# A first pass that goes by pairs of steps, and a SyncE that waits for keys before it loads the fifth weights

## The chip, the cores and the metric

One core of a Trainium2 chip. The metric is the device time of one execution, in microseconds (us); less is better. Five engines work beside each other: PE (TensorE: matmuls), DVE (VectorE), ACT (ScalarE), POOL (GpSimd) and SP (SyncE, which here only starts DMA transfers). ACT starts some transfers as well. Each engine takes its instructions in order, and they wait for each other through semaphores.

## The reference, cut to what matters

```python
# per batch (4) and head (8), D = 48, 768 time steps
cur = outer(u * k_t, v_t)
y_t = r_t @ (state + cur)
state = w_t[:, None] * state + outer(k_t, v_t)
# then, for 3072 tokens of width 384
h = x @ w_in                      # 384 -> 2048
g = h * clip(h + 3, 0, 6) / 6
x = g @ w_out                     # 2048 -> 384
xn = x / rms(x) * rms_g
out = (silu(xn @ w_gate) * (xn @ w_val)) @ w_out2
```

## The kernel before

The attention runs in chunks of 64 time steps, in 24 sets g (a chunk of two batches each). Each set has a cumulative product of decays by a scan (`prep_scan`), its reciprocal (`prep_inv`, in two parts), the scaled keys (`prep_k`) and receptances (`prep_r`), scores, a masked product with the values (`outputs`), new state sums (`sums`) and the part from the older state (`across`). The weights of the first expert layer come from memory as fp32, and are split into a hi part (ACT, `split_up`, L491) and a lo part (POOL, `split_up`, L927), for products of three matmuls in the fast format; the down products of the first pass use the raw fp32 weights (`down_raw`, L1104).

A pass e handles 512 tokens (the passes 0 and 1 handle 256 each) in NF1 = 16 steps f. In step f PE makes `up(e, f)`: nine matmuls into one of two PSUM banks. ACT (`up_gate`, L536) and DVE (`hidden`, L789) turn the bank into g, and PE later multiplies g by the down weight (`down`, L1094), two steps behind. `up(f)` waits until hidden(f - 2) has freed its bank (s_g) and, in pass 0, for the lo part of weight f (s_wloU). The attention of the coming sets lies in these steps by a table written by hand: `half_a` (L260) for pass 0, `cycles` for the others. A set has four phases: MEET (scores of set g + 1, outputs, sums and across of set g), PREP, INV1 and INV2. All engines walk the same table. The order on each engine is the order of the Python program:

- SP (L414 to L453) loads dec, rkn, rkt and weights in a fixed order, with waits before each that frees its buffer. After `load_rk(2)` it goes straight on to the weights 4 and 5 (`FIRST_UP` = 4), then `load_dec(3)`, `load_rkn(3)`, `load_rk(3)`.
- ACT (L665 to L693) copies and fills the bonus of sets 0 and 1 into the attention matrix, copies keys, splits the first weights and copies x1 (`x1_hi`, L524), which waits for `outputs`. In pass 0 each step evacuates `up`, then does attention, a split and the fill of bonus 2.
- DVE (L885 to L910) prepares sets 0 and 1, masks scores, makes x1's lo part, `update_state(0)`, `prep_scan(2)`; then 16 steps of `hidden` and attention.
- POOL (L1012 to L1029): products `rk_mul` and `prep_r` of sets 0 and 1, the lo splits, and `rku_mul(2)` between the second and the third split.
- PE (L1277 to L1294): warm-up matmuls `busy`, bonuses, scores, keys, sums, outputs of sets 0 and 1, then the passes in `run1` (L1219). A semaphore's name tells the maker: s_ki scaled keys, s_kiT transposed keys, s_g g, p_y outputs.

`meet(e, f, g)` on PE is, for a set with state: `scores(g + 1)` (L1129), `outputs(g)` (L1158, from set 2 on), a wait for hidden(f - 1), `sums(g)` (L1150) into two PSUM banks (one of them the up bank that is free) and `across(g)` (L1186, from set 2 on).

Of the kernel before, what the change touches and what calls it, by code (L numbers as in the profile page):

```python
# [40 lines left out]
NF1, NF2 = F1 // P, F2 // P  # L41
# [15 lines left out]
FIRST_UP = 4  # L57
# [10 lines left out]
def build(nc, decT, rkT, valN, rkN, u, u_heads, w_in, w_out, w_gate, w_val, w_out2, rms_g, out, x2_dram):  # L68
    with ExitStack() as ctx:
# [94 lines left out]
        def sum_bank(g, b):  # L164

            if b == 0:
                return ps_c
            return ps_o[2] if g == 0 else ps_h[g == 1]

        s_val0, s_val3, s_rkt, p_bn, s_half, s_last = (sem(n) for n in ("s_val0", "s_val3", "s_rkt", "p_bn", "s_half", "s_last"))  # L170
        ldD = [sem(f"ldD{i}") for i in range(2)]
# [46 lines left out]
        def has_state(g):  # L218

            return g < GROUPS - SETS  # L220
# [12 lines left out]
        def sums_read(eng, g):  # L233

            need(eng, s_state, STATE_INCS * g + 2)
# [14 lines left out]
        MEET, PREP, INV1, INV2 = range(4)  # L250

        def cycles(c):

            steps = {0: [(INV2, c * B - 1)]}
            for b in range(B):
                for phase in (MEET, PREP, INV1, INV2):
                    steps.setdefault(4 * b + 1 + phase, []).append((phase, c * B + b))
            return steps

        half_a = {4: [(MEET, 1)], 6: [(PREP, 1)], 7: [(INV1, 1)], 8: [(INV2, 1)],  # L260
                  9: [(MEET, 2)], 10: [(PREP, 2)], 11: [(INV1, 2)], 12: [(INV2, 2)],
                  13: [(MEET, 3)], 14: [(PREP, 3)], 15: [(INV1, 3)]}

# [83 lines left out]
        def _(sp):  # L347
# [7 lines left out]
            def load_rk(g):  # L355

                need(sp, s_ki, g - 1)
                need(sp, s_rd, g - 1)
                if PLACED <= g < 2 * PLACED:
                    sp.wait_ge(s_rkt, g - 1)  # L360
                for j in (1, 0):
                    sp.dma_start(rkt[HI2 * j:HI2 * j + D, slot(g), :, :, :, :], rkT[g // SETS, g % SETS, j, 0:D]).then_inc(ldR[slot(g)], 16)
# [57 lines left out]
            load_rkn(2)  # L420
            load_dec(2)
            load_rk(2)
            for f in range(FIRST_UP, FIRST_UP + 2):
                load_up(sp, f)
                load_dn(sp, f - 2)
# [54 lines left out]
        def _(act):  # L480
# [10 lines left out]
            def split_up(f):  # L491

                act.wait_ge(ldUp[f], 16)
                act.activation(w_up[:, f, 0, :], raw_up[:, f, 1, :], ACT.Copy).then_inc(s_whiU, 1)
# [6 lines left out]
            def fill_bonus(g, part):  # L501

                q = slot(g)
                if part == 0:
                    act.wait_ge(s_bonus, g + 1)
                    need(act, p_y, g - 1)
                for j in range(2):
                    for p in range(2 * part, 2 * part + 2):
                        last = act.activation(att[:, q, j, p, :], diag[:, :], ACT.Copy, scale=bonus[:, q, 2 * p + j:2 * p + j + 1])
                        last.then_inc(s_fill, 1)  # L510
# [160 lines left out]
                    copy_keys(0)  # L671
            for g in range(2):
                keep_last(g)
            split_up(0)
            x1_hi(0, 0)
            split_up(1)
            x1_hi(1, 0)
            copy_keys(1)
            for f in range(2, FIRST_UP):
                split_up(f)  # L680
            for f in range(NF1):
                up_gate(0, f)
                for phase, g in half_a.get(f, ()):
                    if (phase, g) != (MEET, 1):
                        attention(phase, g, 0)
                if f + FIRST_UP < NF1:
                    split_up(f + FIRST_UP)
                if f in (1, 2):
                    fill_bonus(2, f - 1)
                if f in (1, 4):  # L690
                    keep_last((2, 3)[f // 4])
                if f >= LATE:
                    split_dn(f - LATE)  # L693
# [15 lines left out]
        def _(dve):  # L709
            def prep_scan(g):  # L710

                q = slot(g)
                landed(dve, ldD, g, 2)
                need(dve, s_ki, g - 1)
                need(dve, s_rd, g - 1)
                need(dve, s_last, g - 1)
                dve.tensor_tensor_scan(*(t.rearrange("p a b t -> p (a b t)") for t in (
                    cum[0:DP, q, :, :, :], dec[0:DP, q, :, :, :], first1[0:DP, :, :, :])), 1.0,
                                       ALU.mult, ALU.add).then_inc(s_cum, 1)
# [11 lines left out]
            def prep_k(g):  # L731

                q = slot(g)
                landed(dve, ldR, g, 2)
                dve.wait_ge(s_inv, PAIRS * (g + 1))
                dve.tensor_tensor(*(t.rearrange("p a b t -> p (a b t)") for t in (
                    ki[0:DP, q, :, :, :], rkt[0:DP, q, 1, :, :, :], ki[0:DP, q, :, :, :])), ALU.mult).then_inc(s_ki, 1)
# [31 lines left out]
            def sum_bonus(g):  # L769

                dve.wait_ge(s_rku, g + 1 - PLACED)
                need(dve, s_fill, H * (g - 1))
                dve.tensor_reduce(bonus[:, slot(g), :], rkn[:, slot(g), 0, :].rearrange("p (h d) -> p h d", h=H),
                                  AX_X, ALU.add).then_inc(s_bonus, 1)
# [118 lines left out]
            for g in range(2):  # L893
                x1_lo(g, 0)
            update_state(0)
            prep_scan(2)
            for f in range(NF1):
                hidden(0, f)
                if f == 0:
                    sum_bonus(2)  # L900
                if f < 2:
                    prep_inv(2, f)
                if f == 2:
                    prep_k(2)
                if f == 3:
                    prep_scan(3)
                for phase, g in half_a.get(f, ()):
                    attention(phase, g, 0)
                if f in (4, 5):
                    prep_inv(3, f - 4)  # L910
# [15 lines left out]
        def _(pool):  # L926
# [27 lines left out]
            def rk_mul(g):  # L954

                landed(pool, ldR, g, 2)
                r_in, k_in = (rkt[0:DP, g, i, :, :, :].rearrange("p a b t -> p a (b t)") for i in range(2))
                pool.tensor_tensor(rk_t[g][0:DP, :, :], r_in, k_in, ALU.mult).then_inc(s_rkt, 1)

            def prep_r(g):  # L960

                q = slot(g)
                landed(pool, ldR, g, 2)
                pool.wait_ge(s_cum, g + 1)
                need(pool, p_y, g - 1)
                pool.tensor_tensor(*(t.rearrange("p a b t -> p (a b) t") for t in (
                    rd[0:DP, q, :, :, :], rkt[0:DP, q, 0, :, :, :], cum[0:DP, q, :, :, 0:T])), ALU.mult).then_inc(s_rd, 1)
# [43 lines left out]
            pool.memset(val3[:, :, :, :, :], 0.0).then_inc(s_val0, 1)  # L1011
            rk_mul(0)  # L1012
            prep_r(0)
            prep_r(1)
            rk_mul(1)
            for f in range(2):
                split_up(f)
            pool.wait_ge(ldU, 16 * PB)
            rku_mul(2)
            for f in range(2, FIRST_UP):  # L1020
                split_up(f)
            prep_r(2)
            for f in range(NF1):
# [17 lines left out]
        def _(pe):  # L1041
# [40 lines left out]
            def up(e, f, par):  # L1082
                need(pe, s_g, e * NF1 + f - 1)
                if e == 0:
                    pe.wait_ge(s_wloU, f + 1)
                if (e, f) == (0, 1):
                    pe.wait_ge(s_kiT, 2)
                dst = ps_h[f % 2][:, tokens(e)]
                if f == 0:
                    first_hidden(dst, w_up[:, f], par, tokens(e), B // 2 if e == 0 else B * e).then_inc(p_up, 1)  # L1090
                else:
                    into_hidden(dst, w_up[:, f], par, tokens(e)).then_inc(p_up, 1)
# [114 lines left out]
            def meet(e, f, g):  # L1207

                if g + 1 < GROUPS:
                    scores(g + 1)  # L1210
                if g >= PLACED:
                    outputs(g)
                if has_state(g):
                    pe.wait_ge(s_g, e * NF1 + f)
                    sums(g)
                if g >= PLACED:
                    across(g)

            def run1(e, par, steps, norm=None):  # L1219

                for f in range(NF1):
                    for phase, g in steps.get(f - 1, ()):
                        if phase == MEET and has_state(g):
                            sums_read(pe, g)
                    if e in (1, 2) and f == 0:
                        down(e - 1, NF1 - 2)
                    up(e, f, par)
                    for phase, g in steps.get(f, ()):
                        if phase == MEET:
                            meet(e, f, g)  # L1230
                        if phase == INV1 and has_state(g + 1):
                            keys(g + 1)
                    if (e, f) == (0, 2):
                        sums_read(pe, 0)
                    if f >= 2:
                        down(e, f - 2)
                    elif e and (f == 1 or e > 2):
                        down(e - 1, NF1 - 2 + f)
                    if norm:
                        norm(f)  # L1240
# [41 lines left out]
            scores(0)  # L1282
            keys(0)
            busy(3)
            pe.wait_ge(s_bonus, 1)
            sums(0)
            bonuses(1)
            busy(4)
            scores(1)
            outputs(0)  # L1290
            outputs(1)
            pe.wait_ge(s_bonus, PLACED)
            keys(1)
            run1(0, 0, half_a)  # L1294
            run1(1, 0, cycles(1))
            for c in range(2, NCH):
                run1(c, (c - 1) % 2, cycles(c))
# [82 lines left out]
```

## Time and profile before

| | us |
|---|---|
| median of 3 runs | 935.19 (935.14 to 936.35) |
| the profiled execution | 934.01 |
| its span in the trace | 932.3 |
| PE busy | 919.8 (99%) |
| DVE, ACT, POOL busy | 518.8, 362.0, 293.2 |

The profile is of one execution, 1.2 us below the median of the runs. Times in it count from the start of the span. A row of the timeline gives the start, the length, the engine, the line of the kernel, the operation, what it writes and reads, how many instructions were merged, and in brackets how long the engine had been idle before it and what released it. An SPq row is a DMA issue by SP. The clock column (PEclk) is the share of TensorE's full clock that was granted, 1.00 for 2.4 GHz and 0.50 for 1.2 GHz.

### The profile page before, as it was taken

To read this page: it belongs to the slowest core of one execution; us is meant where nothing else is said; L and a number is where in the kernel's file an instruction comes from. 1 tells how busy PE (TensorE), PEld (TensorE's weight loads), DVE (VectorE), ACT (ScalarE), POOL (GpSimd) and SP (SyncE) were. 2 spreads that over 40 slices of the span, in tenths; PEclk is the share of its full clock that TensorE was granted. 3 is DMA by queue.
4 is the path that set the end of the run, shared out by engine and by line. 5 is a ranking of instruction groups with operands and counts; after the bars stand their busy time and mean duration, and the time that the engine had idled before them with its cause. 6 is when DMAs were issued, how large, how long until landed. Compare 5 with 4: busy or idle time off the path is not lost.

```text
span 932.3 us, 17546 instructions
## 1 busy us (share of the span) xinstructions
PE 919.8 (99%) x7064; PEld 772.9 (83%) x7064; DVE 518.8 (56%) x752; ACT 362.0 (39%) x786; POOL 293.2 (31%) x244
## 2 busy tenths in 40 slices
PE   7999999999999999999999999999999999999998
PEld 6899988888888888888888888888888888888887
DVE  5998976666656666314874553553463373363332
ACT  4556554454444444336563123123223223223212
POOL 3888645454445445324341011011011001101000
PEclk9999999999999999999999999999999999999999
DMA  9774442233223321014321010000010001000000
GB/s 257 231 207 128 118 130 61 69 98 96 66 62 106 80 72 52 20 40 134 88 88 38 1 35 34 1 34 34 0 34 35 1 25 44 0 1 34 1 1 34
DMA packets 33008, 60.40 MB, mean 65 GB/s; under 512 B 6112, under 2 KB 19936, under 8 KB 32928
## 3 DMA queue, kind: packets, MB, share of 16 engines
q1 hardware_dynamic: 27104, 50.82, 18.9%
q10 hardware_dynamic: 5824, 8.47, 3.1%
q8 instruction: 56, 0.92, 0.4%
q14 instruction: 24, 0.20, 0.1%
HBM read 47.66 MB, written 9.44 MB: 61 GB/s over the span
## 4 chain that ended last, share of the span: by engine, by line
PE 96%; issue 1%; DVE 1%; ACT 1%; POOL 1%; SPq 0%; DMA 0%; DVEq 0%; ACTq 0%; POOLq 0%
PE acc L1076 35%; PE bank L1047 12%; PE bank L1049 12%; PE bank L1048 12%; PE pair L1049 5%; PE pair L1048 5%; PE pair L1047 5%; PE acc L1110 2%; PE pair L1129 1%; PE pair L1186 1%; PE pair L1158 1%; PE bank L1150 1%; PE bank L1065 1%; PE acc L1275 1%; PE bank L1139 1%
## 5 line engine op out<-in xcount | busy, mean ns | idle before, releaser
L1076 PE MATMUL acc<-gs,w_dn 128*128 128x512 f32 (+1 forms) x1512 | 357.0, 382 | 0.2 <-issue 0.2
L1076 PEld LDWEIGHTS acc<-gs,w_dn 128*128 128x128 f32 x1512 | 273.0, 188 | 54.0 <-issue 0.3
L943 POOL TENSOR_TENSOR gs<-act_g,gs 128x512 fp32r<-128x512 f32 (+1 forms) x96 | 121.7, 1268 | 205.3 <-ACT gs L549 205.1
L1047 PE MATMUL bank<-xs,w_up 128*128 128x512 f32 (+1 forms) x459 | 172.0, 375 | 1.5 <-POOL w_up L930 1.4
L1049 PE MATMUL bank<-xs,w_up 128*128 128x512 f32 (+1 forms) x459 | 169.0, 368 | 0.0
L1048 PE MATMUL bank<-xs,w_up 128*128 128x512 f32 (+1 forms) x459 | 169.0, 368 | 0.0
L799 DVE SCALAR_TENSOR_TENSOR act_g<-act_u,bank 128x512 f32<-128x512 f32 (+1 forms) x112 | 67.5, 602 | 137.9 <-ACT act_u L541 137.8
L867 DVE TENSOR_TENSOR act_u<-act_u,bank 128x512 f32<-128x512 f32 x72 | 49.5, 688 | 146.8 <-ACT act_u L611 146.8
L541 ACT ACTIVATE act_u<-bank,half 128x512 f32<-128x512 f32 (+1 forms) x112 | 70.1, 626 | 154.1 <-PE bank L1049 144.5
L615 ACT ACTIVATE gs<-act_g 128x512 fp32r<-128x512 f32 x72 | 45.5, 632 | 155.9 <-DVE act_g L873 155.9
L611 ACT ACTIVATE act_u<-bank 128x512 f32<-128x512 f32 x72 | 43.1, 598 | 149.0 <-PE bank L1049 149.0
L1047 PEld LDWEIGHTS bank<-xs,w_up 128*128 128x128 f32 x459 | 86.4, 188 | 16.8 <-issue 1.6
L1048 PEld LDWEIGHTS bank<-xs,w_up 128*128 128x128 f32 x459 | 86.5, 188 | 14.8
L1049 PEld LDWEIGHTS bank<-xs,w_up 128*128 128x128 f32 x459 | 86.4, 188 | 14.6
L989 POOL TENSOR_TENSOR xs<-ntmp,xs 128x512 fp32r<-128x512 f32 x18 | 26.1, 1448 | 225.8 <-ACT xs L574 225.8
L729 DVE RECIPROCAL ki<-cum 112x128 f32<-112x128 f32 x96 | 84.2, 921 | 0.8
L549 ACT ACTIVATE gs<-act_g 128x512 fp32r<-128x512 f32 (+1 forms) x96 | 57.2, 596 | 65.9 <-DVE act_g L799 65.3
L873 DVE TENSOR_TENSOR act_g<-act_u,pair 128x512 f32<-128x512 f32 x72 | 49.6, 688 | 51.9 <-PE pair L1049 51.2
L877 DVE TENSOR_TENSOR gs<-act_g,gs 128x512 fp32r<-128x512 f32 x72 | 55.3, 768 | 36.8 <-ACT gs L615 36.3
L1047 PE MATMUL pair<-xs,w_up 128*128 128x512 f32 x144 | 56.0, 389 | 0.0
L1048 PE MATMUL pair<-xs,w_up 128*128 128x512 f32 x144 | 56.0, 389 | 0.0
L1049 PE MATMUL pair<-xs,w_up 128*128 128x512 f32 x144 | 56.0, 389 | 0.0
(121 smaller groups left out, 1121.2 us busy)
## 6 DMA issues: line engine op xcount, KB each, us to landing
rkn<-in_rkN SPq DMA_DIRECT2D x22, 384.0 KB, 4.2
rkt<-in_rkT SPq DMA_DIRECT2D x44, 192.0 KB, 3.7
val<-in_valN SPq DMA_DIRECT2D x22, 256.0 KB, 3.0
x<-x_dram SPq DMA_DIRECT2D x6, 768.0 KB, 4.3
dec<-in_decT SPq DMA_DIRECT2D x46, 97.5 KB, 2.3
x_dram<-xo SPq DMA_DIRECT2D x5, 768.0 KB, 4.1
out<-xo SPq DMA_DIRECT2D x5, 768.0 KB, 3.3
raw_dn<-in_w_out SPq DMA_DIRECT2D x14, 192.0 KB, 5.2
```

Of the source, the lines that this page charges most:

```text
L541: act.activation(act_u[:, f % 2, tok], ps_h[f % 2][:, tok], ACT.Relu, scale=1.0 / 6.0, bias=half[:, 0:1]).then_inc(s_u, 1)
L549: act.activation(gs[:, f % GRING, 0, tok], act_g[:, f % 2, tok], ACT.Copy).then_inc(s_ghi, 1)
L729: dve.reciprocal(ki[0:DP, q, p, :, :], cum[0:DP, q, p, :, 1:T1]).then_inc(s_inv, 1)
L799: dve.scalar_tensor_tensor(out=g_of(e, f), in0=act_u[:, f % 2, tok], scalar=1.0, in1=ps_h[f % 2][:, tok], op0=ALU.min, op1=ALU.mult).then_ ...
L867: dve.tensor_tensor(act_u[:, f % 2, :], act_u[:, f % 2, :], ps_h[f % 2][:, :], ALU.mult).then_inc(s_silu, 1)
L873: dve.tensor_tensor(act_g[:, f % 2, :], act_u[:, f % 2, :], ps_v[f % 2][:, :], ALU.mult).then_inc(s_h, 1)
L877: dve.tensor_tensor(gs[:, f % GRING, 1, :], act_g[:, f % 2, :], gs[:, f % GRING, 0, :].bitcast(F32), ALU.subtract).then_inc(s_hlo, 1)
L943: pool.tensor_tensor(gs[:, f % GRING, 1, tok], act_g[:, f % 2, tok], gs[:, f % GRING, 0, tok].bitcast(F32), ALU.subtract).then_inc(s_glo, 1)
L1047: pe.matmul(dst, w_hi, x_hi, start=first, stop=False)
L1048: pe.matmul(dst, w_hi, x_lo, start=False, stop=False)
L1049: last = pe.matmul(dst, w_lo, x_hi, start=False, stop=end)
L1076: last = pe.matmul(ps_o[m][:, tok], w[:, wp, m * P:(m + 1) * P], gs[:, f % GRING, xp, tok], start=f == 0 and a == 0, stop=f == nf - 1 and ...
```

## The change

SP waits for the scaled keys of set 1 (s_ki 2) before it starts the loads of weights 4 and 5 and all behind them. Pass 0 gets a PE function of its own: two ups, then (from the second pair on) two downs; the meeting of set 1 moves from step 4 to step 5, so that meetings are at 5, 9 and 13 and the sums use the same up bank each time. In the start, `bonuses(1)` goes ahead of `sums(0)` on PE; on POOL `rk_mul(1)` goes ahead of `prep_r(1)`, behind a wait for the scan of set 1, and three splits instead of two stand ahead of `rku_mul(2)`; on ACT the second split goes ahead of `x1_hi(0)` and the third between the two `x1_hi`; bonus 2 is filled in steps 2 and 3 instead of 1 and 2. On DVE `prep_scan(2)` goes behind `hidden(0)` and `sum_bonus(2)` from step 0 to step 2.

```diff
--- before.py
+++ after.py
@@ -165,7 +165,7 @@
 
             if b == 0:
                 return ps_c
-            return ps_o[2] if g == 0 else ps_h[g == 1]
+            return ps_o[2] if g == 0 else ps_h[0]
 
         s_val0, s_val3, s_rkt, p_bn, s_half, s_last = (sem(n) for n in ("s_val0", "s_val3", "s_rkt", "p_bn", "s_half", "s_last"))
         ldD = [sem(f"ldD{i}") for i in range(2)]
@@ -257,7 +257,7 @@
                     steps.setdefault(4 * b + 1 + phase, []).append((phase, c * B + b))
             return steps
 
-        half_a = {4: [(MEET, 1)], 6: [(PREP, 1)], 7: [(INV1, 1)], 8: [(INV2, 1)],
+        half_a = {5: [(MEET, 1)], 6: [(PREP, 1)], 7: [(INV1, 1)], 8: [(INV2, 1)],
                   9: [(MEET, 2)], 10: [(PREP, 2)], 11: [(INV1, 2)], 12: [(INV2, 2)],
                   13: [(MEET, 3)], 14: [(PREP, 3)], 15: [(INV1, 3)]}
 
@@ -420,6 +420,7 @@
             load_rkn(2)
             load_dec(2)
             load_rk(2)
+            sp.wait_ge(s_ki, 2)
             for f in range(FIRST_UP, FIRST_UP + 2):
                 load_up(sp, f)
                 load_dn(sp, f - 2)
@@ -671,12 +672,13 @@
                     copy_keys(0)
             for g in range(2):
                 keep_last(g)
-            split_up(0)
+            for f in range(2):
+                split_up(f)
             x1_hi(0, 0)
-            split_up(1)
+            split_up(2)
             x1_hi(1, 0)
             copy_keys(1)
-            for f in range(2, FIRST_UP):
+            for f in range(3, FIRST_UP):
                 split_up(f)
             for f in range(NF1):
                 up_gate(0, f)
@@ -685,8 +687,8 @@
                         attention(phase, g, 0)
                 if f + FIRST_UP < NF1:
                     split_up(f + FIRST_UP)
-                if f in (1, 2):
-                    fill_bonus(2, f - 1)
+                if f in (2, 3):
+                    fill_bonus(2, f - 2)
                 if f in (1, 4):
                     keep_last((2, 3)[f // 4])
                 if f >= LATE:
@@ -893,14 +895,14 @@
             for g in range(2):
                 x1_lo(g, 0)
             update_state(0)
-            prep_scan(2)
             for f in range(NF1):
                 hidden(0, f)
                 if f == 0:
-                    sum_bonus(2)
+                    prep_scan(2)
                 if f < 2:
                     prep_inv(2, f)
                 if f == 2:
+                    sum_bonus(2)
                     prep_k(2)
                 if f == 3:
                     prep_scan(3)
@@ -1011,13 +1013,14 @@
             pool.memset(val3[:, :, :, :, :], 0.0).then_inc(s_val0, 1)
             rk_mul(0)
             prep_r(0)
+            pool.wait_ge(s_cum, 2)
+            rk_mul(1)
             prep_r(1)
-            rk_mul(1)
-            for f in range(2):
+            for f in range(3):
                 split_up(f)
             pool.wait_ge(ldU, 16 * PB)
             rku_mul(2)
-            for f in range(2, FIRST_UP):
+            for f in range(3, FIRST_UP):
                 split_up(f)
             prep_r(2)
             for f in range(NF1):
@@ -1216,25 +1219,39 @@
                 if g >= PLACED:
                     across(g)
 
-            def run1(e, par, steps, norm=None):
-
-                for f in range(NF1):
-                    for phase, g in steps.get(f - 1, ()):
-                        if phase == MEET and has_state(g):
-                            sums_read(pe, g)
-                    if e in (1, 2) and f == 0:
-                        down(e - 1, NF1 - 2)
-                    up(e, f, par)
-                    for phase, g in steps.get(f, ()):
-                        if phase == MEET:
-                            meet(e, f, g)
-                        if phase == INV1 and has_state(g + 1):
-                            keys(g + 1)
-                    if (e, f) == (0, 2):
+            def step(e, f, par, steps):
+
+                for phase, g in steps.get(f - 1, ()):
+                    if phase == MEET and has_state(g):
+                        sums_read(pe, g)
+                up(e, f, par)
+                for phase, g in steps.get(f, ()):
+                    if phase == MEET:
+                        meet(e, f, g)
+                    if phase == INV1 and has_state(g + 1):
+                        keys(g + 1)
+
+
+            def first_pass():
+
+                for f in range(0, NF1, 2):
+                    step(0, f, 0, half_a)
+                    step(0, f + 1, 0, half_a)
+                    if f == 2:
                         sums_read(pe, 0)
                     if f >= 2:
+                        down(0, f - 2)
+                        down(0, f - 1)
+
+            def run1(e, par, steps, norm=None):
+
+                for f in range(NF1):
+                    if f == 0 and e < 3:
+                        down(e - 1, NF1 - 2)
+                    step(e, f, par, steps)
+                    if f >= 2:
                         down(e, f - 2)
-                    elif e and (f == 1 or e > 2):
+                    elif f == 1 or e > 2:
                         down(e - 1, NF1 - 2 + f)
                     if norm:
                         norm(f)
@@ -1282,16 +1299,16 @@
             scores(0)
             keys(0)
             busy(3)
+            bonuses(1)
             pe.wait_ge(s_bonus, 1)
             sums(0)
-            bonuses(1)
             busy(4)
             scores(1)
             outputs(0)
             outputs(1)
             pe.wait_ge(s_bonus, PLACED)
             keys(1)
-            run1(0, 0, half_a)
+            first_pass()
             run1(1, 0, cycles(1))
             for c in range(2, NCH):
                 run1(c, (c - 1) % 2, cycles(c))
```

## Rows read from the trace of the kernel before

**Rows 1.** The page: part 1 (engines) and part 3 (DMA queues).
```profile
PE 919.8 (99%) x7064; PEld 772.9 (83%) x7064; DVE 518.8 (56%) x752; ACT 362.0 (39%) x786; POOL 293.2 (31%) x244
...
q8 instruction: 56, 0.92, 0.4%
```

**Rows 2.** Busy time by stretch: PE, PEld, DVE, ACT, POOL, PEclk, DMA share, GB/s.
```profile
13.10:19.10 6.00, 4.01 (x124) 3.69 (x125) 4.02 (x6) 3.51 (x15) 1.51 (x2) 1.00 1.07 274
...
17.70:21.70 4.00, 0.00 (x0) 0.00 (x0) 0.73 (x1) 0.92 (x5) 0.99 (x1) 0.97 1.07 299
...
21.70:24.90 3.20, 3.15 (x59) 2.92 (x59) 1.26 (x3) 1.81 (x4) 1.60 (x2) 0.50 1.06 244
...
28.30:69.90 41.60, 41.56 (x549) 38.32 (x550) 38.44 (x58) 23.76 (x70) 34.66 (x31) 1.00 0.73 215
...
46.00:46.70 0.70, 0.70 (x5) 0.60 (x4) 0.70 (x1) 0.70 (x5) 0.70 (x1) 1.00 0.27 89
```

**Rows 3.** Timeline of PE, 20 to 29 us: start, length, engine, line, what.
```profile
21.75 0.37 PE L1165 MATMUL pair<-att,val 64*64 64x64 f32 x3 [4.07 <-issue]
...
28.34 0.36 PE L1047 MATMUL bank<-xs,w_up 128*128 128x256 f32 x1 [1.44 <-POOL w_up L930]
```

**Rows 4.** DMA queues in 19.1 to 20.2 us: packets, MB, share.
```profile
q8 instruction: 1, 0.02, 6.2%
```

**Rows 5.** The chain that ended last, in order of time: start, length, what.
```profile
13.59 0.22 PE bank L1150
...
35.01 0.45 PE bank L1150 x28
...
35.46 1.49 PE acc L1110 x6
...
38.03 1.30 PE acc L1110 x6
...
47.89 0.62 PE pair L1129 x32
...
67.27 2.61 PE acc L1110 x12
```

**Rows 6.** Timeline of SP, a DMA issue.
```profile
13.31 0.43 SPq L320 DMA_DIRECT2D raw_up<-in_w_in  x1
```

**Rows 7.** DMA queues in 46.6 to 47.7 us.
```profile
q8 instruction: 1, 0.02, 5.7%
```

**Rows 8.** Timeline of DVE, 15 to 36 us.
```profile
15.17 0.69 DVE L736 TENSOR_TENSOR ki<-rkt,ki 112x512 f32<-112x512 f32 x1
...
25.20 1.23 DVE L717 TENSOR_TENSOR_SCAN cum<-dec,first 112x520 f32<-112x520 f32 x1
...
26.38 0.42 DVE L799 SCALAR_TENSOR_TENSOR act_g<-act_u,bank 128x256 f32<-128x256 f32 x1
...
27.27 0.55 DVE L773 TENSOR_REDUCE bonus<-rkn 128x8 f32<-128x384 f32 x1 [0.47 <-POOL rkn L952]
...
27.74 0.94 DVE L729 RECIPROCAL ki<-cum 112x128 f32<-112x128 f32 x1
...
28.88 2.56 DVE L729 RECIPROCAL ki<-cum 112x128 f32<-112x128 f32 x3
...
33.05 2.69 DVE L717 TENSOR_TENSOR_SCAN cum<-dec,first 112x520 f32<-112x520 f32 x1
```

**Rows 9.** Timeline of ACT, 22 to 33 us.
```profile
22.32 0.49 ACT L530 ACTIVATE xs<-pair 128x384 fp32r<-128x384 f32 x1 [3.71 <-PE pair L1165]
...
30.07 0.51 ACT L494 ACTIVATE w_up<-raw_up 128x384 fp32r<-128x384 f32 x1
...
30.48 1.05 ACT L509 ACTIVATE att<-diag,bonus 128x64 f32<-128x64 f32 x4
...
32.06 0.47 ACT L541 ACTIVATE act_u<-bank,half 128x256 f32<-128x256 f32 x1 [0.53 <-PE bank L1049]
```

**Rows 10.** Timeline of POOL.
```profile
24.26 1.02 POOL L950 TENSOR_TENSOR rkn<-rkn 128x384 f32<-128x384 f32 x1
```

More of the change, by code:

```diff
@@ L1217, in meet @@
                     across(g)
+            def step(e, f, par, steps):
[13 more added lines that the diff above has]
+                    if f == 2:
+                        sums_read(pe, 0)
+                    if f >= 2:
+                        down(0, f - 2)
+                        down(0, f - 1)
             def run1(e, par, steps, norm=None):
                 for f in range(NF1):
-                    for phase, g in steps.get(f - 1, ()):
-                        if phase == MEET and has_state(g):
-                            sums_read(pe, g)
-                    if e in (1, 2) and f == 0:
+                    if f == 0 and e < 3:
                         down(e - 1, NF1 - 2)
-                    up(e, f, par)
-                    for phase, g in steps.get(f, ()):
-                        if phase == MEET:
-                            meet(e, f, g)
-                        if phase == INV1 and has_state(g + 1):
-                            keys(g + 1)
-                    if (e, f) == (0, 2):
-                        sums_read(pe, 0)
+                    step(e, f, par, steps)
                     if f >= 2:
                         down(e, f - 2)
-                    elif e and (f == 1 or e > 2):
+                    elif f == 1 or e > 2:
                         down(e - 1, NF1 - 2 + f)
```

## The prediction

> **What bounds the kernel now.** I read the page first: TensorE (PE) is busy 99% of the span [rows 1], so time can only come out of a hole in PE or of work taken from it, and the change takes no matmul away. The stretches come next [rows 2]. From 28.3 to 69.9 us, the rest of the first pass, PE works 41.56 of 41.60 us. Before it stand 4 us without any PE work (17.7 to 21.7) and 3.2 us at a granted clock of 0.50, the lower level, 1.2 GHz; the clock fell after PE had stood still for nearly four microseconds.
>
> PE's own timeline names the hole [rows 3]: it stops inside `outputs(0)`, with three matmuls of line 1165 to go, for 4.07 us, and the releaser is "issue". No semaphore is waited for there. The instruction queue of PE moved 56 packets of 16 KB [rows 1]; 7064 matmuls and as many weight loads over 56 are some 252 instructions a packet. One such packet moved in 19.1 to 20.2 [rows 4], and 1.5 us after its end PE went on. So I read the hole as a late block of instructions. PE had run some 456 by then; it enters the block before the missing one near instruction 200, which is the start of `sums(0)` at 13.59 [rows 5], and that is when the next can be asked for. It moved 5.5 us later, with the DMA engines full (1.07 from 13.1 to 19.1 [rows 2]). By 13.3 SP had issued u_b, rkn, dec and rkt, then from 13.31 on [rows 6] weights, dec(3), rkn(3) and rkt(3). At the other end of the scale a packet went in 46.6 to 47.7 [rows 7], just after the DMA share had been 0.27 [rows 2]: there PE has no pause that the views put forward.
>
> **Part 1: SP waits for s_ki 2, then loads the fifth weights.** `prep_k(1)` ends at 15.86 [rows 8], so the loads from 13.31 start some 2.6 us later. Queued behind the wait on SP: up weights 4 and 5 and down weights 2 and 3, dec, rkn and rkt of set 3, then up 6 and down 4, up to `load_val(2)`, where SP stood anyway until `outputs(0)` was done, at about 22; that slack covers the shift. Late next is the fifth hi/lo split, which PE wants only at step 4. Cost: nothing. Gain: if packets are served in the order in which they are asked for, the fetch now finds only what was issued by 13.3. From 13.1 to 19.1 the engines moved 274 GB/s [rows 2], 1.64 MB. What SP had issued by 13.3 and had hardly begun is u_b, rkn, dec and rkt of set 2, by their shapes in the code 1.15 MB, 4.2 us at that rate: they are through at 17.3, and the packet can go then instead of at 19.1. So the pause ends near R = 19.9 in place of 21.75, and a little sooner as the bonus stands earlier: I take R = 19.8; bounds 17.7 (no pause) and 21.75. A pause of 2.1 us need not drop the clock; I take full clock.
>
> **Part 2: bonuses(1) first on PE, rk_mul(1) first on POOL, splits regrouped.** The bonus moves ahead of `sums(0)` and `fill_bonus(1)` ends about 1.3 us earlier, but that lies in front of the pause and is worth nothing while the pause stands. The third weight's lo part no longer waits behind `rku_mul(2)`: the 1.44 us that PE waited for it ahead of 28.34 [rows 3] goes, if nothing else is late. I price that with the next part, since something else is.
>
> **Part 3: pairs of steps.** On PE they save nothing: a down is 1.30 between two ups, and two downs side by side took 2.61 [rows 5]. They ask for more sooner: up 3 comes before any down, and the meeting at 5 needs `hidden(4)` only one up after up 4.
>
> **Part 4: the scan of set 2 goes behind hidden(0).** This is where I expect the start's gain to be eaten. VectorE (DVE) does, in order: scan(2), a reciprocal, hidden(1), three reciprocals, hidden(2), sum_bonus(2); then ScalarE (ACT) fills, evacuates up 3, splits a weight, fills again, evacuates up 4; then DVE does hidden(4), for which `sums(1)` waits. From the scan's end [rows 8, 9]: 0.94 + 0.40 + 2.56 + 0.38 + 0.55 = 4.83; 1.05 + 0.47 + 0.51 + 1.05 + 0.47 = 3.55; 0.4; ten hand-overs at 0.04: together 9.2. Then the sums and downs 2 and 3: before, sums at 35.01 to the end of down 2 at 36.95 and 1.30 for down 3, 3.24 [rows 5]. So six ups and four downs are done at scan end + 12.5 (0.05 for the hand-over). Before, that point was 38.03 + 1.30 = 39.33 [rows 5]. Gain = 26.8 - scan end.
>
> When does the scan end? Before, `hidden(0)` began 4.63 after R (26.38 - 21.75) [rows 3, 8]. With PE at full clock some 1.4 of its 3 us in between go (half of the rest of the outputs and of up 0), and the split that ACT now does between the two x1 copies adds 0.5 [rows 9]: R + 3.7, ended at R + 4.1. POOL meanwhile: x1_hi(0) at R + 0.4 and 0.49 long, the split 0.51, then lo(2) 1.0 to R + 2.45, two multiplications at 1.02 to R + 4.5, lo(3) to R + 5.5 [rows 9, 10]. Scans took 1.23 and 2.69 us [rows 8]; the long one began in a stretch of POOL instructions back to back. So the scan either goes in at R + 4.5 (end R + 5.65) or behind the next split (R + 6.65). With R = 19.8 it ends at 25.45 to 26.45: gain 1.35 to 0.35, I take the middle, 0.9. PE alone would be there 3 us sooner, so the freed PE time mostly turns into waiting for s_g at up 3, up 5 and the sums of the meeting.
>
> **Part 5: the meeting at 9.** It stands 12 PE instructions (one down) earlier in the stream. A block boundary lies just ahead of it now, the next just before its end: a meeting is four groups of 32 weight loads and matmuls like the scores' 0.62 us [rows 5], some 2 us, and a fetch takes 1.1 us on its queue and 1.5 until PE goes on [rows 3, 4], plus its start. Before, the packet in 46.6 to 47.7 [rows 7] came just in time. Now the distance is 2.3 us in place of 2.7: cost 0.15 at least; up to 1.8 if the fetch falls behind the decays and rkt loads, as the first one did. I take 0.3. The bank swap (`sum_bank` to bank 0) and sums_read cost nothing: two downs, 2.6 us, lie between the meeting and the next up.
>
> Behind the first pass the instructions are the same, and PE is 99% busy, so the shift is carried to the end. Sum: 0.9 - 0.3 = 0.6 us off the profiled execution: 934.01 to 933.4. The median of the runs is 935.19, 1.2 above the profiled one; so 934.6.
>
> **Rivals.** (A) The fetch is in time and there is no pause. For it: the moved bonus and the wait both help, and one fetch at low DMA load was prompt. Against it: the 1.15 MB of u_b, rkn, dec and rkt issued by 13.3 are still moving until about 17. POOL then binds: from 17.7 three splits at 1.0, two multiplications, a split and the scan: its end is 24.95, or 23.9 if it goes ahead of the last split. Gain 1.85 to 2.9, less 0.3: 933.1 (932.6 to 933.7). Should the DVE chain be shorter than I make it, PE's own bound adds up to 1.5 more, 931.8.
>
> (B) Slower: the fetch does not queue behind SP's loads, and the delay does not move it; R stays at 21.75. With the clock at half, hidden(0) ends at 26.8 as before, but the scan, which was over at 26.43, now ends at 28.05 to 28.5. Gain 26.8 - 28.3 = -1.5, and 0.3 at the meeting: 937.0 (936.3 to 938.7). It decides from R above 20.9, where 26.8 - (R + 6.15) falls below -0.3. For it: that the packet waited behind data is read off one fetch. Against it: the 5.5 us under load, and no visible delay at 46.6.
>
> The Trainium skill, DMA: Bandwidth & Descriptors, "Queues, rings and completion order", says that each DMA engine takes turns between the queues it has work for; by that rule a lone instruction packet would never wait for a long data queue, rival B would hold, and the forecast would be 937.0. The 5.5 us of rows 4 and 5 speak against it here. The Trainium skill, Runtime: NRT & Kernel Launch, "Instruction fetch mechanics", calls the cost of crossing a block mostly hidden; the 4.07 us of rows 3 is not hidden, if my reading is right.
>
> (C) The change does nothing, as `s_ki` 2 is long there when SP comes: excluded, 13.31 is before 15.86.
>
> **How the numbers follow.** Forecast 0.50, A 0.30, B 0.20. A measurement can tell 0.2%, 1.9 us. Of A about nine tenths with its longer tail lie beyond 933.3, of the forecast a tenth (scan early and R near 18.5): faster 0.32. Of B more than half lies beyond 937.1, of the forecast's tail (the meeting's fetch at 1.8, and stalls at the meetings at 9 and 13 on hidden(8) and hidden(12)) some 0.07: slower 0.19. The rest, 0.49, is no difference. The range goes from A's shorter chain, 931.8, to B, 937.2.
>
> **What would show it.** PE's gap inside `outputs(0)` ends near 19.8, with no stretch at clock 0.50; the instruction packet moves near 17.2. SP's `raw_up` issue is at 15.9. PE waits for DVE's hidden (L799) before up 3 and before line 1150 of the meeting at 5; the scan of set 2 ends at 25.4 to 26.5; down 3 ends near 38.4. A small issue gap stands in the meeting at 9. I am wrong if the gap still ends after 21, if it is gone, or if PE works from up 2 to the meeting without waits; then the time is B's, A's, or below 932.

## The result, and the profile after

The change makes the kernel slower: 938.37 us median of 18 runs (933.6 to 940.45) against 935.16 of 18 runs of the kernel before (931.88 to 936.73), ratio 1.0036 with a 95% interval of 1.0026 to 1.0046. That is 3.2 us more where I forecast 0.6 less, and above my range. Single executions differ by 4.9 us (the kernel before) and 6.9 us (the changed one), so only medians and intervals over many runs are compared below, and a trace is read for its waits.

The profiled execution of the changed kernel took 938.00 us, 4.0 more than that of before. Its page, engines and clock (answering to [rows 1]):

```profile
PE 922.8 (99%) x7064; PEld 775.1 (83%) x7064; DVE 519.0 (55%) x752; ACT 361.7 (39%) x786; POOL 293.0 (31%) x244
...
PEclk7999999999999999999999999999999999999999
```

Busy time by stretch (columns as in [rows 2]):

```profile
12.00:22.00 10.00, 10.00 (x182) 9.67 (x184) 5.78 (x9) 6.05 (x24) 4.38 (x4) 0.50 1.05 280
...
43.00:48.00 5.00, 3.77 (x84) 3.27 (x82) 4.97 (x5) 2.41 (x9) 3.30 (x3) 1.00 0.39 140
```

What PE waited for, over the whole span (engine and line, releaser: total us, times, longest):

```profile
PE bank L1153 <- DVE act_g L801: 3.0, 2, 1.6
...
PE acc L1079 <- issue: 1.5, 1, 1.5
...
PE bank L1050 <- DVE act_g L801: 1.4, 2, 1.1
...
PE acc L1177 <- POOL xo L960: 1.4, 1, 1.4
```

The chain that ended last at two points (answering to [rows 5]), the end of down 3 and of down 14:

```profile
35.34 2.79 PE acc L1113 x12
...
68.81 3.90 PE acc L1113 x18
```

The timelines of ACT and DVE (answering to [rows 8, 9]; L719 is the scan, L775 sum_bonus):

```profile
25.25 1.23 DVE L719 TENSOR_TENSOR_SCAN cum<-dec,first 112x520 f32<-112x520 f32 x1
...
39.13 0.52 ACT L495 ACTIVATE w_up<-raw_up 128x384 fp32r<-128x384 f32 x1 [4.10 <-DMA raw_up<-in_w_in]
...
42.81 0.55 DVE L775 TENSOR_REDUCE bonus<-rkn 128x8 f32<-128x384 f32 x1 [2.34 <-POOL rkn L954]
...
44.55 2.85 DVE L719 TENSOR_TENSOR_SCAN cum<-dec,first 112x520 f32<-112x520 f32 x1
...
57.20 3.84 DVE L719 TENSOR_TENSOR_SCAN cum<-dec,first 112x520 f32<-112x520 f32 x1
```

Read in order: six ups and four downs are done at 35.34 + 2.79 = 38.13; before it was 39.33, so the start has gained 1.2 us. Down 14, the first pass's fifteenth down, ends at 68.81 + 3.90 = 72.71, before at 67.27 + 2.61 = 69.88 [rows 5]: 2.8 us behind. So 4 us are lost between down 3 and down 14. Two waits of PE before the sums (L1153), 3.0 us in all, stand there, 1.62 in the meeting at 9 and 1.33 in the one at 13, and 0.3 before up 9. Counted from start to start they weigh a little more: the sums began 2.26 and 1.98 us behind the start of the outputs where it was 0.46 before, 3.3 us more in all, and up 9 some 0.5 us late. Behind down 14 a block of instructions came 1.5 us late, near 92 us (0.2 at the same place before), and from there on the changed kernel is 4.0 us behind, to the end.

Ahead of the sums DVE is never idle (4.97 of the 5 us from 43 to 48). Behind the wait stands `hidden`, behind that the scan: 2.85 and 3.84 us, where the shortest take 1.23. Before, the same two scans took 2.27 and 1.71:

```profile
43.65 2.27 DVE L717 TENSOR_TENSOR_SCAN cum<-dec,first 112x520 f32<-112x520 f32 x1
...
56.26 1.71 DVE L717 TENSOR_TENSOR_SCAN cum<-dec,first 112x520 f32<-112x520 f32 x1
```

This is what POOL did during the long one of the changed kernel:

```profile
56.37 1.62 POOL L968 TENSOR_TENSOR rd<-rkt,cum 112x512 f32<-112x512 f32 x1
...
57.95 1.01 POOL L939 TENSOR_TENSOR w_dn<-raw_dn,w_dn 128x384 fp32r<-128x384 f32 x1
...
58.92 1.02 POOL L932 TENSOR_TENSOR w_up<-raw_up,w_up 128x384 fp32r<-128x384 f32 x1
...
59.90 1.93 POOL L939 TENSOR_TENSOR w_dn<-raw_dn,w_dn 128x384 fp32r<-128x384 f32 x1
```

Four instructions with hardly a gap. The scan was issued at 57.20 and ended at 61.04: if its own 1.23 us stand at the end, they began near 59.8, so it let the current POOL instruction and two more go by. That is worked out from the rows; the trace doesn't show the inside of a scan. The first of the two waits has another cause ahead of its scan: ACT stood 4.10 us for the raw tenth weight (39.13), POOL's `rku_mul(3)` was queued behind that weight's lo split, and DVE stood 2.34 us for it (42.81).

### The profile page after: what moved, and what is told of

The parts are those of the page before. It is cut to its first block, busy times and chain, and to the rows that moved or that the text cites. A ratio compares the mean times of both kernels' runs of the same rounds, so it can differ in the third digit from the quotient of the medians.

```text
span 936.3 us, 17547 instructions
## 1 busy us (share of the span) xinstructions
PE 922.8 (99%) x7064; PEld 775.1 (83%) x7064; DVE 519.0 (55%) x752; ACT 361.7 (39%) x786; POOL 293.0 (31%) x244
## 4 chain that ended last, share of the span: by engine, by line
PE 94%; DVE 3%; issue 1%; ACT 0%; POOL 0%; SPq 0%; DMA 0%; DVEq 0%; POOLq 0%; ACTq 0%
PE acc L1079 35%; PE bank L1050 11%; PE bank L1051 11%; PE bank L1052 11%; PE pair L1051 5%; PE pair L1052 5%; PE pair L1050 5%; PE acc L1113 2%; PE pair L1132 1%; PE pair L1189 1%; DVE cum L719 1%; PE pair L1161 1%; PE bank L1153 1%; PE bank L1068 1%; PE bank L1142 1%
## 5 line engine op out<-in xcount | busy, mean ns | idle before, releaser
L1050 PE MATMUL bank<-xs,w_up 128*128 128x512 f32 (+1 forms) x459 | 171.0, 373 | 1.6 <-DVE act_g L801 1.4
L1050 PEld LDWEIGHTS bank<-xs,w_up 128*128 128x128 f32 x459 | 86.4, 188 | 17.4 <-DVE act_g L801 2.3
L1050 PE MATMUL pair<-xs,w_up 128*128 128x512 f32 x144 | 56.0, 389 | 0.0
```

The source lines that it names most:

```text
L1050: pe.matmul(dst, w_hi, x_hi, start=first, stop=False)
```

## The experiments

Every kernel was timed in five rounds against the kernel before on the same chip: 12 runs of each and 35 of the kernel before. The first four kernels ran on one chip, the next four on a second, the last four on a third, so kernels of different groups are compared by their ratios to the kernel before.

**Is it the pairs?** The changed kernel with the old first pass (`run1(0, 0, half_a)`, meeting 1 at step 4):

```diff
-            first_pass()
+            run1(0, 0, half_a)
```

> The changed kernel with the old first pass (one up, one down, meetings at 4, 9, 13); start and SP wait stay changed. Theory P (the pairs lose the time: the sums of the meetings at 9 and 13 wait for the hidden of the up just before, 1.62 and 1.33 us in the changed kernel's trace): those two waits fall under 0.3 us each and the median comes back by some 3 us, to about the kernel before or 1 us below it. Theory S (the start or the SP wait loses it, through the low clock at the start and late instruction blocks): no move, still 2.5 to 3.5 us above the kernel before.

Ratio 0.999 (0.9975 to 1.0006), median 934.29: the loss is gone, and the two waits too (0.4 us is left in the meeting at 4). Then the kernel before with only the pairs:

```diff
-            run1(0, 0, half_a)
+            first_pass()
```

> The kernel before with only the first pass by pairs (and its meeting at 5 and bank); old start, no SP wait. Theory P: slower than before by 2.5 to 4.5 us, with waits of 1 us and more before the sums of the meetings at 9 and 13, and the 4 us pause inside outputs(0) as before. Theory S: within 1 us of the kernel before.

Ratio 1.0038 (1.0021 to 1.0054). The pairs carry the whole loss. The traced execution was the fastest of the twelve (934.84 us, median 937.82), and its pause was 2.6 us long and not 4. PE's waits there, the first row the two meetings, the second the pause of the start:

```profile
PE bank L1150 <- DVE act_g L799: 2.8, 2, 1.5
...
PE pair L1165 <- issue: 2.6, 1, 2.6
```

**Is it the SP wait?** The kernel before with that one line:

> The kernel before with only the SP wait for s_ki 2. If the instruction fetch queues behind SP's loads (my forecast), the pause inside outputs(0) ends near 19.9 instead of 21.75 or is gone, and the time falls by 1.5 to 4 us, since the old first pass has slack on DVE. If the fetch does not queue there (rival B of the prediction), the pause still ends at 21.5 to 22 and the time is that of the kernel before within 0.5 us.

Ratio 0.9994 (0.9977 to 1.0012), median 932.75 against 934.11: a gain of 0.6 us by the ratio, 1.4 by the medians, which the runs don't prove and which is less than the 1.5 to 4 expected. In its trace the pause is 1.0 us long and ends at 20.4, between what the two theories said, and more waits stand elsewhere:

```profile
PE bank L1048 <- POOL w_up L931: 2.1, 1, 2.1
...
PE pair L1166 <- issue: 1.0, 1, 1.0
...
PE pair L1187 <- issue: 0.8, 1, 0.8
```

The third lo part is 2.1 us late at up 2. The pause had begun later, since part of the start ran at a granted clock of 0.50. So the pause is not the clean quantity that one trace made of it.

**Do the sums wait only for want of a down ahead of them?** `step` gets one more argument, a down that it does between the up and the meeting:

```diff
-                    step(0, f + 1, 0, half_a)
+                    meets = f + 1 in (5, 9, 13)
+                    step(0, f + 1, 0, half_a, f - 2 if meets else None)
...
-                        down(0, f - 2)
+                        if not meets:
+                            down(0, f - 2)
                         down(0, f - 1)
```

> The changed kernel, but in the pairs with a meeting one of the two downs is done ahead of the meeting (up, up, down, meeting, down). Theory P: the waits of 1.62 and 1.33 us before the sums shrink by the length of a down, 1.30 us, to 0.3 or less; the median falls by 2 to 3 us against the changed kernel. Theory S: no move.

Ratio 1.0031 (1.0014 to 1.0047), median 937.75: no repair. The wait moves behind the meeting, to the up that needs the state updated (L1050):

```profile
PE bank L1050 <- DVE state L762: 2.5, 4, 0.9
...
PE bank L1153 <- DVE act_g L801: 0.7, 2, 0.4
```

The waits before the sums fell from 3.0 to 0.7 as this theory said, and 0.66 us came up behind each of the two meetings (two of the four waits of the first row). DVE is as late as in the changed kernel, and what changed is mainly where PE meets it. So moving a down ahead of the meeting does not cure it: of the 3.0 us of waits 2.0 are left, the time moved by 0.5 us, which the runs can't tell from nothing, and my 2 to 3 us were a miss.

**What makes DVE late?** POOL steps aside for the scans:

```diff
             for f in range(NF1):
+                if f in (7, 11, 15):
+                    pool.wait_ge(s_cum, f // 4 + 4)
                 if f + FIRST_UP < NF1:
```

> The changed kernel, but POOL waits at the start of steps 7, 11 and 15 until DVE's scan of that step is done, so that it does not hold the port that both share. Theory P1 (the pairs make POOL's instructions stand back to back, the scans of sets 4 and 5 starve, 2.85 and 3.84 us in the changed kernel where 1.23 is the time alone, and the sums of the meetings wait for the hidden behind them): both scans fall to 1.2 to 1.9, the waits of 1.62 and 1.33 before the sums fall under 0.5 each, the median falls by 2 to 3 us. Theory P2 (the sums wait since up 8 and 12 are only one up old, whatever the scans take): scans shorter, waits stay above 1 us, no gain.

Ratio 0.9993 (0.9976 to 1.001), median 934.51: the loss is gone by this alone. DVE's rows, sum_bonus(3), scan(4) and scan(5):

```profile
39.30 0.55 DVE L775 TENSOR_REDUCE bonus<-rkn 128x8 f32<-128x384 f32 x1 [2.29 <-POOL rkn L954]
...
41.02 1.89 DVE L719 TENSOR_TENSOR_SCAN cum<-dec,first 112x520 f32<-112x520 f32 x1
...
52.71 1.88 DVE L719 TENSOR_TENSOR_SCAN cum<-dec,first 112x520 f32<-112x520 f32 x1
```

1.88 in place of 3.84, and 1.89 in place of 2.85. The meeting at 13 has no wait. The one at 9 keeps 0.65, as sum_bonus(3) still came late behind POOL: its scan is 0.96 us shorter and its wait 0.97 us, so here the wait follows the scan one for one. By the ratios the kernel gained 4.0 us, more than the 2 to 3 expected. The trace is of its fastest execution, so its start is not typical. Next the late weight:

```diff
-                if s == 2:
+                if s == 3:
                     load_rk(4)
                     load_rkn(4)
-                if s == 3:
                     load_dec(5)
```

> The changed kernel, but SP issues the rkt and rkn loads of set 4 behind the tenth up weight (step 3) and not before it (step 2). Theory P3 (the pairs want the tenth weight sooner, it lands late, ACT stands 4.1 us for it, POOL's rku_mul of set 3 is behind it and DVE's sum_bonus waits 2.34 us): the ACT wait falls under 1 us, the DVE wait too, the wait before the sums of the meeting at 9 goes, the one at 13 stays (1.3): 1 to 1.6 us less. Theory P1: ACT's wait falls, the scans stay at 2.8 and 3.8, no more than 0.7 us less.

Ratio 1.0020 (1.0007 to 1.0033), median 937.23, 1.5 us less than the changed kernel by the ratios, as P3 said, though the two intervals overlap. ACT's wait for the tenth weight and DVE's for POOL are gone, scan(4) takes 1.89, and one of the two waits before the sums with it; scan(5) still starves, and the meeting at 13 waits 1.3:

```profile
41.84 1.89 DVE L718 TENSOR_TENSOR_SCAN cum<-dec,first 112x520 f32<-112x520 f32 x1
...
54.58 3.85 DVE L718 TENSOR_TENSOR_SCAN cum<-dec,first 112x520 f32<-112x520 f32 x1
```

```profile
PE pair L1167 <- issue: 2.5, 1, 2.5
...
PE bank L1152 <- DVE act_g L800: 1.3, 1, 1.3
```

Both edits:

> Both edits together on the changed kernel. P1 and P3 each: no wait above 0.3 us before the sums of both meetings, the median within 1 us of the kernel before or under it, 3 us under the changed kernel.

Ratio 0.997 (0.9953 to 0.9987), median 932.88 against 935.47: the lowest ratio of the study, and the only one whose interval lies below 1. No wait for DVE before the sums is left, with the order of the pairs unchanged, which speaks against P2. By the ratios it is 6 us under the changed kernel where 3 were expected. Two kernels below that differ from it in one part lie at 0.999 and 1.0008, so part of its lead may be chance. What is left is mostly late instructions, and 1.2 us before two ups of the second pass for a state that DVE updates:

```profile
PE pair L1169 <- issue: 3.0, 1, 3.0
...
PE acc L1080 <- issue: 1.3, 1, 1.3
```

**The start.** The kernel before with the new order of the start alone:

> The kernel before with only the new order of the start (bonuses, splits, scan and sum_bonus of set 2), no SP wait, no pairs. If the start is what costs 1.2 us near 91 us of the span (a late instruction block, in all three kernels so far with the new start and in none with the old): the gap stands there again, and the time is 0.5 to 1.5 us above that of the kernel with the SP wait alone. If that gap is chance, it is not there.

Ratio 0.9996 (0.998 to 1.0011). The late block near 91 us was there (1.5 us), the median 935.36 against 935.47. The new start costs nothing that the runs can show: the kernel with the SP wait alone had 0.9994. Then the pause itself, with SP's queue kept empty ahead of it:

```diff
+            sp.wait_ge(s_ki, 2)
             load_rkn(2)
             load_dec(2)
             load_rk(2)
```

> The kernel before, with SP's wait for s_ki 2 ahead of load_rkn(2), so that rkn, dec and rkt of set 2 too are issued only after 15.9: the SP queue is empty between u_b and then. If the instruction packet queues behind SP's data (theory F), it goes by 15.5, as ACT's loads are through at 14, and the 4 us pause inside outputs(0) is gone (under 0.5 us). If its time has nothing to do with SP's loads (theory G), the packet goes at 17.4 to 19.1 as in all but one of the traces so far, and the pause stays at 1 us or more. The total can be worse either way, as set 2's data come 3 to 5 us late.

In 15.0 to 16.4 us the instruction queue shows its packet:

```profile
q8 instruction: 1, 0.02, 4.3%
```

and PE has no pause in `outputs(0)` that is put down to issue. The packet started at 15.05; in twelve of the other thirteen traces it started between 16.98 and 19.11, after SP's queue had moved 1.1 to 1.6 MB from 13 us on. That fits a fetch that queues behind SP's data, but it is one trace, and there is one against it: in the trace of the kernel where POOL yields, with all of set 2's loads issued by 13.3, the packet started at 14.03. So theory F is likely and not proven.

That the pause is a late packet stands on more. In all eleven traces with a pause, PE went on 1.2 to 1.6 us after the end of the packet. Of the three without one, two have the packets of 14.03 and 15.05; in the third, the changed kernel's, PE ran at half clock and came to the missing instructions no sooner than they were there.

But the time is that of before (1.0002, 0.9983 to 1.002), since PE's waits are now of other kinds:

```profile
PE bank L1151 <- DVE act_g L800: 2.3, 1, 2.3
...
PE bank L1048 <- POOL w_up L931: 1.8, 1, 1.8
...
PE acc L1077 <- issue: 1.3, 1, 1.3
...
PE acc L1159 <- DVE att L744: 1.0, 1, 1.0
```

**Taking the parts out of the best kernel.**

> Both repairs (POOL yields to the scans, rkt and rkn of set 4 behind the tenth weight) on the changed kernel, without the SP wait for keys. If the SP wait is worth what the kernel with the wait alone hinted at (about 1 us in the mean), this is 0.5 to 1.5 us above the kernel with both repairs and the wait, at 0.998 to 0.999 of the kernel before; if it is worth nothing, at 0.997.

Ratio 1.0008 (0.9989 to 1.0027): without the SP wait the repaired kernel is no faster than the one before. With it 0.997, on another chip: 3.6 us between the two, more than the 0.5 to 1.5 expected, but the intervals nearly touch (0.9987 and 0.9989), and the traces show no shorter pause with the wait (3.0 us) than without it (2.3), so its size is open.

> Pairs, SP wait and both repairs, but the old order of the start. If the new start brings the late block near 91 us of the span (1.17 to 1.55 us, in five of six traces with the new start, in none with the old), that gap is under 0.3 us here, and the time is at or below the one with the new start, 0.995 to 0.997 of the kernel before; the 1.4 us wait for the third lo part ahead of up 2 comes back.

Ratio 0.999 (0.9972 to 1.0009), median 932.28 against 934.73. My guess on the late block was wrong: it is there with the old start too (0.9 us, L1078), and in the next kernel, again with the old start (1.45 us). It is not the start's. (The count in the expectation was off as well: by then the block was late in six of seven traces with the new start, by 0.90 to 1.55.)

```profile
PE bank L1049 <- POOL w_up L930: 2.1, 1, 2.1
...
PE pair L1167 <- issue: 1.5, 1, 1.5
...
PE acc L1078 <- issue: 0.9, 1, 0.9
```

> The kernel before with the SP wait and both repairs, no pairs, old start. If pairs bring nothing even when repaired, this is as fast as the repaired pairs or faster, 0.996 to 0.998 of the kernel before. If pairs are worth something once DVE is not held, this is about 1 us slower than the repaired pairs, 0.998 to 1.0.

Ratio 0.9998 (0.998 to 1.0016), median 933.7 against 934.73. Paired and single passes can't be told apart once DVE is not held up.

## Why the prediction was wrong, step by step

- **What bounds the kernel; the pause is a late block of instructions**: right. PE went on 1.2 to 1.6 us after the packet in all eleven traces with a pause, and where the packet started at 14.03 and 15.05 there was none.
- **Part 1, R = 19.8**: the term was mis-sized, by taking one execution for the kernel before. I set 19.8 against 21.75. Over all four traces without the SP wait the pause ended between 19.9 and 21.75, in the seven with it at its place that had a pause between 19.6 and 21.1: 20.6 and 20.4 in the mean, so 0.3 us and not 1.95. The packet itself started at 17.9 in the mean without the wait and at 17.6 with it, the one of 14.03 left out. That what lies ahead of the fetch in either case is the data issued by 13.3 fits these numbers and is not shown. "I take full clock" was wrong too: in all eleven traces with a pause the clock stood at 0.50 for 3.4 or 6.8 us in the start, also where the pause was only 1.9 us long. Two traces with the wait have no pause. In the changed kernel's own, PE ran at half clock from 12 to 22 and did not get ahead of its instructions; before the clock fell it had waited 1.4 us for POOL (L1177). "Late next is the fifth split" was wrong: the tenth was.
- **Part 3, what the pairs cost**: here the forecast failed. The sum has a term for the start and one for a late block, and none for the sums of the meetings at 9 and 13. I wrote that the meeting at 5 needs `hidden(4)` early and priced that one; the same need at 9 and 13 I left to a tail of 0.07, without following DVE behind step 5. The scans of sets 4 and 5 stand there, 2.85 and 3.84 us long. How long a scan takes is not its own: it holds what POOL leaves free. I had the 2.69 us row before me, read it rightly as starving, and applied it only to the scan of set 2. In the pairs the ups, and with them ACT's splits, come in twos, and DVE reaches its scan while POOL has four instructions queued; that the twos are the reason is my reading, that POOL's company is the cost is shown by the first repair. That cost 3.0 us of waits before the sums, 3.3 from start to start, and the pairs alone made the kernel slower by 0.38%.
- **Part 4, the scan of set 2 behind hidden(0)**: the number was right, the way to it was not. The scan ended at 26.48 (forecast 25.4 to 26.5) and PE waited 1.1 us for `hidden(1)` before up 3. But I had the scan ready at 23.9 and held up by POOL; it was ready only at 25.3, as PE had run at half clock, and then took the shortest time of all, 1.23 us. The wait that I expected before the sums of the meeting at 5 did not come. So the end of down 3, 38.13 and within 0.3 us of the 38.4 I gave, is luck in good part.
- **Part 5, a late block in the meeting at 9**: not there. Its length, 1.5 us, turned up at 92 us, for a reason that stays open.
- **The rivals**: B lies nearest by its time, 937.0, but its loss was to come in the start, and there the changed kernel gained 1.2 us. The half of B that says that the delay does not move the packet comes near what the traces show. A has its sign, no pause, in the profiled execution, but not its reason (the fetch was not in time, PE was slow), and not its time of 933.1. The loss that came, a DVE that POOL keeps waiting ahead of the meetings at 9 and 13, was no rival of mine.

The Trainium skill, SBUF — State Buffer, "Who interferes with whom", says that a DVE instruction with two SBUF inputs and a GpSimd instruction that reads SBUF exclude each other, and that the order of issue decides. The traces agree as to the exclusion (1.23 us at the shortest, 3.84 in the company above). They show more than that: by the rows above, a scan that was waiting was passed over at two POOL instruction boundaries.

What stays open: why the block near 91 us is late by 0.9 to 1.5 us in ten of the fourteen traces, and by 0.2 or less in the other four; whether the packet of the start queues behind SP's data; and how much the SP wait is worth alone.

## What to carry to other kernels

A duration read in a trace belongs to its neighbourhood: where two engines keep each other waiting, as DVE's scan and POOL do here, take the shortest one as the work and the rest as waiting, and ask what the new order puts beside it. When PE is 99% busy, an order that lets it run ahead in bursts may make the helpers work in bursts too; a semaphore wait on the engine that can spare the time gave back 4 us here (1.0036 to 0.9993). And one trace of a start is one draw: the pause ended anywhere from 19.6 to 21.75, and in three of the fourteen traced executions it was not there.

## What the runs showed of the hardware that I had not expected

- A scan of DVE (112 x 520 fp32, two SBUF inputs) took from 1.23 to 3.85 us by what POOL did. The longest let two more POOL instructions go first; in others DVE came in at the first boundary (the 1.71 of before). A wait on POOL cut 2.85 and 3.84 to 1.89 and 1.88.
- The instruction block that PE lacked in the start began to move between 17.0 and 19.1 us in twelve traces, at 14.03 in one with the same loads of SP issued, and at 15.05 with SP's queue empty. PE went on 1.2 to 1.6 us after its end.
- The granted clock fell to 0.50, 1.2 GHz, within the first 40 us in thirteen of the fourteen traces, once for 10 us (12 to 22) while PE was issuing small matmuls all the time, after 1.4 us of standing still; in one trace (the first repair's, 930.12 us) it stayed at 1.00 until the last microseconds.
- Much of the spread between executions goes with that clock. Of the 105 executions of the kernel before that stand beside the experiments, the ten with a mean granted clock of 1.000 took 930.8 us in the mean, the other 95 took 934.9; the three fastest of the changed kernel (933.6, 934.11, 935.26) are its three at 1.000. Which is the cause, the clock or the pause, these runs don't tell.
